# Order of the transposes of x and of the attention weights on TensorE and ScalarE in a fused attention and two-MoE kernel

## What is computed

```
# attention, B=4, H=8, S=576, head_dim=64, k = 32
scores = (q @ k.T) / sqrt(64)
kth    = np.partition(scores, -32, axis=-1)[..., -32:-31]
attn   = softmax(where(scores >= kth, scores, -1e9))
x      = (attn @ v)  ->  rows of 2304 tokens x 512
# soft MoE, 8 experts with 4 slots each
logits = x @ phi                      # 2304 x 32
slot_input = softmax(logits, axis=0).T @ x;  slot_out = relu(slot_input @ w1) @ w2
x      = softmax(logits, axis=1) @ slot_out
# noisy top-2 MoE over 8 experts, added up in out
```

## Time and profile before

| | us |
|---|---|
| median of 3 runs (lowest, highest) | 1099.03 (1091.27, 1117.39) |
| the profiled execution | 1102.3 |
| its span in the trace | 1100.5 |
| TensorE busy | 964.0 (88%) |
| VectorE busy | 782.9 (71%) |
| ScalarE busy | 624.8 (57%) |
| POOL busy | 619.0 (56%) |

### The profile page before, as it was taken

How to read it: one execution, slowest core, us unless ns; L and a number is a source line. 1 busy time by engine, 2 the same in 40 slices (tenths; PEclk the granted TensorE clock), 3 DMA queues, 4 the chain that set the end, 5 groups by cost and what they waited for, 6 DMA issues and landing times.

```text
span 1100.5 us, 20957 instructions
## 1 busy us (share of the span) xinstructions
PE 964.0 (88%) x6238; PEld 682.0 (62%) x6238; DVE 782.9 (71%) x1515; ACT 624.8 (57%) x1269; POOL 619.0 (56%) x936
## 2 busy tenths in 40 slices
PE   3898988988988988988988988996699999999995
PEld 1566666656655665665666666432377777777784
DVE  6999999998989989989889887204734433444341
ACT  2788887787777868777678776202323332333221
POOL 3577776766767757767667664101435444454553
PEclk9999999998999989999899899999889999999998
DMA  9910110110110110110201002899914435433332
GB/s 353 418 32 24 67 45 14 55 46 13 55 46 2 67 27 19 67 29 19 67 13 33 13 6 107 340 422 422 425 28 113 97 55 117 110 47 41 38 38 36
DMA packets 25011, 109.07 MB, mean 99 GB/s; under 512 B 3360, under 2 KB 4832, under 8 KB 17760
## 3 DMA queue, kind: packets, MB, share of 16 engines
q1 hardware_dynamic: 17040, 87.82, 20.9%
q0 software_dynamic: 7168, 11.21, 8.0%
q10 hardware_dynamic: 720, 8.98, 2.2%
HBM read 88.39 MB, written 16.07 MB: 95 GB/s over the span
## 4 chain that ended last, share of the span: by engine, by line
PE 33%; DVE 22%; issue 17%; POOL 12%; DMA 9%; ACT 5%; POOLq 1%; DVEq 0%; SPq 0%; ACTq 0%
PE psum L965 11%; PE psum L627 7%; POOL arena L1549 7%; PE psum L970 5%; DVE arena L1238 5%; DVE arena L1222 4%; DVE arena L1226 4%; DMA out<-arena 3%; DVE arena L1234 3%; DMA arena<-xs_rows,arena 3%; DMA arena<-w_top 2%; PE psum L584 2%; POOL arena L1582 2%; DVE arena L1230 2%; ACT h_hi L1198 2%
## 5 line engine op out<-in xcount | busy, mean ns | idle before, releaser
L1549 POOL TENSOR_SCALAR arena<-arena 128x576 bf16<-128x576 f32 x144 | 249.9, 1735 | 178.5 <-DVE arena L1222 173.6
L627 PE MATMUL psum<-arena 128*128 128x130 f32 x1550 | 226.9, 290 | 30.3 <-ACT arena L1034 30.3
L627 PEld LDWEIGHTS psum<-arena 128*128 128x128 f32 x1550 | 190.4, 188 | 66.9 <-issue 34.5
L584 PE MATMUL psum<-arena 64*128 64x288 f32 (+1 forms) x640 | 117.7, 468 | 55.0 <-DVE arena L1230 50.3
L1226 DVE MAX8 arena<-psum 128x8 f32<-128x576 f32 x144 | 109.4, 760 | 55.8 <-PE psum L596 55.5
L965 PE MATMUL psum<-w_hi,h_hi 128*128 128x512 f32 x320 | 133.6, 418 | 7.1 <-ACT h_hi L1198 2.6
L1508 DVE COPY arena<-psum 128x512 f32 x41 | 28.4, 692 | 156.7 <-PE psum L970 133.7
L993 ACT ACTIVATE arena<-arena 128x576 bf16<-128x576 bf16 x144 | 98.6, 685 | 59.0 <-POOL arena L1549 58.9
L1198 ACT ACTIVATE h_hi<-psum 128x512 fp32r<-128x512 f32 x80 | 43.5, 595 | 154.2 <-PE psum L952 154.1
L965 PE MATMUL psum<-w_lo,h_hi 128*128 128x512 f32 x320 | 129.4, 404 | 0.0
L987 ACT COPY arena<-psum 128x576 f32<-128x576 f32 x144 | 91.0, 632 | 38.3 <-PE psum L584 36.9
(11 more groups left out here) (240 smaller groups left out, 1629.2 us busy)
## 6 DMA issues: line engine op xcount, KB each, us to landing
weights<-w_soft SPq DMA_DIRECT2D x21, 1024.0 KB, 16.7
arena<-qkv SPq DMA_DIRECT2D x15, 864.0 KB, 4.5
weights<-w_top SPq DMA_DIRECT2D x12, 1024.0 KB, 25.8
arena<-w_soft SPq DMA_DIRECT2D x11, 1024.0 KB, 8.1
weights<-w_top SPq DMA_DIRECT2D x3, 2048.0 KB, 27.0
weights<-w_top ACTq DMA_DIRECT2D x3, 2048.0 KB, 10.2
arena<-qkv SPq DMA_DIRECT2D x16, 325.0 KB, 2.9
out<-arena SPq DMA_DIRECT2D x1, 4864.0 KB, 18.0
```

The source lines that it names most:

```text
L584: last = nc.tensor.matmul(bank(2 * (t % 2) + x, SH)[q0:q0 + rows, :], qT[u][half, w * P + q0:w * P + q0 + rows], kT[u][half, h * SH:(h + 1 ...
L627: last = nc.tensor.matmul(o_place(n, k)[0:rows, :], wT[0:kr, t % 2, kc, q0:q0 + rows], v_, start=(kc == 0), stop=(kc == KC - 1))
L1549: nc.gpsimd.tensor_scalar(hit[t % 2], s_sb[t % S_SLOTS], m8[t % S_SLOTS][:, 7:8], None, ALU.is_ge) \
```

## The change

`x_work` is cut in two. The transposes of x in steps 2, 6 and 7 become `x_turn`, which stands ahead of `trans` in TensorE's list, right behind the strike of the second tile of the step before. The products with phi stay where they were, behind `keep_warm`. On ScalarE `x_copy_t`, with its copies of logits in steps 8 and 0, moves from behind `copy_b` to ahead of `wt_a`.

```diff
+                if n == 8:
+                    hold(pe, xt_c, 3 * j + 3)
+                    rest_logits(j, odd)
+
+            def x_turn(now, half, n):
+
+                if isinstance(now, int) and now == 0:
+                    return
+                j, odd = now - 1, 1 - half
                 if n in X_STEPS:
                     pe.wait_ge(o_copied, DPI * now + n - LAG_O + 1)
                     if n == 2:
...
                         hold(pe, x_done, DPI * j + 12)
                         (x_trans(odd, 1, 7) if n == 6 else rest_trans(odd, 7))
-                if n == 8:
-                    hold(pe, xt_c, 3 * j + 3)
-                    rest_logits(j, odd)
...
-            steps(pe, [(0, qk_a), (1, strike_b), (LAG_T, trans), (LAG_O, keep_warm), (None, x_work), (0, qk_b),
+            steps(pe, [(0, qk_a), (1, strike_b), (None, x_turn), (LAG_T, trans), (LAG_O, keep_warm), (None, x_work), (0, qk_b),
                        (0, strike_a), (None, x_taken), (LAG_O, attn_v)])
...
-            steps(act, [(0, copy_a), (1, count_b), (LAG_T, wt_a), (LAG_T, wt_b), (0, count_a), (0, copy_b),
-                        (None, x_copy_t), (LAG_K, exp_a), (LAG_K, exp_b), (LAG_K, below_a), (LAG_K, below_b),
+            steps(act, [(0, copy_a), (1, count_b), (None, x_copy_t), (LAG_T, wt_a), (LAG_T, wt_b), (0, count_a),
+                        (0, copy_b), (LAG_K, exp_a), (LAG_K, exp_b), (LAG_K, below_a), (LAG_K, below_b),
                         (LAG_O, copy_o)])
```

## The result

| | before | changed |
|---|---|---|
| median of the runs, us | 1107.89 (4 runs, 1091.27 to 1117.39) | 1062.03 (4 runs, 1059.73 to 1063.03) |
| the profiled execution | 1102.3 | 1061.45 |
| its span | 1100.5 | 1059.6 |

The ratio to the kernel before is 0.9695, 95% interval 0.963 to 0.976. The change is faster by 2.4 to 3.7%. A second comparison gave 1061.83 us and 0.9645 (0.9585 to 0.9705).

What follows compares the result with a forecast made beforehand. The attention was taken to go at VectorE's pace, its idle time being what can be won. Stalls, clock falls and the move's cost gave 1102.3 - 27.0 - 15.8 + 1.5 = 1061.0 us, range 1050 to 1082.

Steps and rivals of the forecast that it cites:

- Stalls, 27.0 us: VectorE's second MAX8 in steps transposing x: quiet waits for TensorE's strike vanish, 6 x 4.02 + 2.84 = 27.0 us gained.
- Clock falls, 15.8 of 18.1 us: Attention: seven of eight clock falls at TensorE's idle ahead of the product with V go, 15.8 us of 18.1 excess.
- The cost of the move, 1.5 us: ScalarE's weights' copies come later over 21 steps, mostly hidden by its wait for POOL; between 0 and 2 us, taken 1.5.
- Nothing is lost on the way.: Behind the attention: everything following, weight loads included, shifts with its earlier end, so no gain is lost.
- The remaining stalls: VectorE's waits for the strike fall from 47.6 to 3 to 8 us; 2.6 us stand at steps with warming matmuls.
- The runs before: Kernel before: runs from 1091 to 1117 us suggest that the number of clock falls differs between them.
- The wait moves to ScalarE: Rival: weights' copies late, then scores' copy and VectorE's first MAX8; 13.9 us given back, half the falls stay, 1080; chance 0.10.
- the margin of 0.02 to 0.18 us: ScalarE's small weights' copy would end only 0.02 to 0.18 us before POOL's hits at 471.42.
- No change: Rival: late weights' copies hold the product with V as long as the x copy does now; 1099 us, chance 0.06.
- slower: Rival: TensorE and ScalarE wait on each other in a loop, stalls stay plus 13.9 to 18 us; 1116 to 1120, chance 0.04.
- falls stay: Rival: stalls go but TensorE still runs at 1.2 GHz now and then; 1077 us, from 1069 to 1080, chance 0.14.

Runs made afterwards that it cites:

- kernel with the idle filled: Kernel before, with five useless matmuls added in TensorE's idle ahead of the product with V, waits for the x copy left; 1085.22 us, ratio 0.9819.
- ScalarE's half alone: Kernel before with only ScalarE's copy of x moved ahead of the weights' copies, TensorE's order as before; 1078.75 us, ratio 0.9731.
- TensorE's half alone: Kernel before with only TensorE's transposes of x moved early, ScalarE's copy still behind its second scores copy; 1114.56 us, ratio 0.9943.
- n = 2 put back: Kernel with x copied between weights' copies and count, TensorE as before, but step 2's copy again behind the second scores copy; 1078.22 us, ratio 0.9819.
- two useless matmuls: Kernel before, with two matmuls without a use added in TensorE's idle ahead of the product with V; 1083.13 us, ratio 0.9851.

## Why the prediction was right

1061.0 us were predicted and 1062.03 measured, and on the profiled execution, against which the sum was made, 1061.45. Point by point:

- **Stalls, 27.0 us.** Right in mechanism and size. All 21 waits went, and TensorE's 30.3 us of waits for the copy are 0. The kernel with the idle filled has them alone, and its attention ends 25.5 us behind the changed one.
- **Clock falls, 15.8 of 18.1 us.** Right that they hang on TensorE's idle, as the kernel with the idle filled shows; all eight went in the attention. The 18.1 held 0.9 us that were no falls: two waits of 0.70 and 0.65 us at the jump back of the loop, counted as excess over 0.25, stand in the changed kernel too (0.69 and 0.63). So the term measured 17.2 us, 1.4 more than I took; the filled kernel says 17.0.
- **The cost of the move, 1.5 us.** Too high. The attention ends 43.65 us earlier and the two terms above make 44.2, so the move cost 0.5 us, 0.3 of it in two new waits of 0.15 for the strike. ScalarE's last copy of the weights starts at 490.57 in a step whose count starts at 491.18, where the estimate had the pause nearly used up. The transposes of x delay those of the weights by 0.44 us ahead of them (487.40 to 487.84), not by the 0.5 to 0.66 that I took from their busy time. The pause for POOL is left at 0.24 us, not near 0.1.
- **"Nothing is lost on the way."** Wrong. 2.7 us came back behind the attention, 2.6 of them in the first stage, where the clock falls at another place than before. They hid the 2.4 us by which the other two terms were too careful (43.65 against 41.3). That the sum came within half a microsecond is luck: three of its parts were 1.0 to 2.7 us off and balanced.
- **The remaining stalls.** 3.8 us, within the 3 to 8 that were given, but their cause, the warming matmuls, was wrong: with two instead of three they stayed. By the trace it is POOL's mask.
- **The runs before.** That their spread goes with the clock is on record: of the runs of the kernel before that enter the ratios of the experiments, 20 in all, the fastest (1090.97 us) had a mean granted clock of 0.978, the slowest (1111.53 us) 0.954, and the clock goes down with the time almost run by run. The number of falls was counted in the one profile only: 8 at 1102.3 us. The runs of the kernels whose profile has no fall in the attention from 100 to 640 us lie 1 to 12 us apart, those of the kernel before 28.
- **The rivals.** "The wait moves to ScalarE" is what half a change does: with ScalarE's list alone VectorE waits 18.7 us for the scores' copy. For the whole change its cover was 1.1 us beyond what the change uses, so it was further off than the margin of 0.02 to 0.18 us said (measured at n = 2 and 6; n = 7 was not tried). "No change" is what the other half does. Of "slower" and of "falls stay" no trace shows anything in the attention.

The Trainium skill (PSUM — Partial Sum Buffer, "Engine vs sequencer instructions") calls ScalarE's queue strict. The trace of ScalarE's half alone agrees: its copies of the weights stand 2.39 us behind a copy of x whose transposes came last. It didn't decide for the change, which moved those transposes too.

## What to carry to other kernels

When a copy frees a shared bank late, look what its engine waits for around it: a pause of about the copy's length ahead of a wait for a third engine is the place for it; here a copy of 0.58 us in a pause of 0.68 left the attention within 1.5 us of the other order. Moving the producer forward gained nothing here while its consumer stayed, and moving the consumer forward alone, to ahead of other work of its queue, built a new wait (18.7 us). And price an idle of TensorE with the clock that it can cost: here 27 us of stalls carried 17 us of clock falls with them.

## What the hardware showed that I had not expected

- In the attention the clock fell to 1.2 GHz behind single idles of TensorE of 1.60 us (seven times in the kernel before, eight in TensorE's half alone, four with n = 2 put back), of 1.28 us (once) and of 1.26 us (once), and not behind every one of that length: 8 times in 21, 9 in 21, 4 in 7. Behind the 18 waits for ScalarE of up to 0.8 us of ScalarE's half alone, the idles of 1.05 us without warming and the 21 waits of up to 1.2 us beside two useless matmuls it never did. It did at both idles of 3.5 us in the attention without warming, and in an idle of 2.27 us at the end of the attention with five useless matmuls.
- Without warming matmuls TensorE's queue waited 3.58 and 3.47 us for issue where the loop jumps back. No other profile has a wait there; that of 2.27 us with five useless matmuls stands behind the loop. One profile each shows them.
- The same code behind the attention took 423.5 to 431.2 us in the thirteen profiles. The clock in its first stage is one part (58.3 us at a full clock, 60.9 at 0.94 in the changed kernel); the rest is open.
